# Zeroing the output in sixteen parts behind the load of expert 0's rows, an end flag read one double sooner on VectorE, and expert counts in four products

## The reference

```
scores = (z @ z^T) / S;  attn = relu(scores)^2;  x = u * (attn @ v)      B=8, S=3072, d=256, d_qk=64
logits = x @ w_gate;     expert = argmax(logits);  gate = softmax(logits)[expert]      E=8
each expert keeps its first 768 rows, in the order of the rows
h = relu(x_kept @ w1[expert]);  y = h @ w2[expert];  out[row] = gate * y   (rows not kept: 0)
```

## Time and profile before

| | |
|---|---|
| time, median of 3 runs | 877.05 us (876.01 to 877.35) |
| the profiled execution: its time | 877.52 us |
| its span in the profile | 875.7 us |
| around the span (877.52 - 875.7) | 1.8 us |
| groups 1 to 18, first to last logits product | 62.1 to 612.9 us |
| experts, first product to last scatter | 620.2 to 875.7 us |
| busy: TensorE, VectorE, ScalarE, GpSimd | 858.0, 635.4, 573.9, 123.4 us |

### The profile page before, as it was taken

One profiled execution on the slowest core, in us unless ns is written; L12 is line 12 of the kernel. 1 busy time (PEld: TensorE's weight loads), 2 busy tenths in 40 slices (PEclk: granted clock), 3 DMA queues, 4 the chain that ended last, 5 costly groups with the idle time before them and its releaser, 6 DMA issues.

```text
span 875.7 us, 22817 instructions
## 1 busy us (share of the span) xinstructions
PE 858.0 (98%) x7293; PEld 684.7 (78%) x7294; DVE 635.4 (73%) x1381; ACT 573.9 (66%) x874; POOL 123.4 (14%) x121
## 2 busy tenths in 40 slices
PE   6999999999999989999999999999999999999997
PEld 5887887888888867888888888888677777777776
DVE  7976777888888968878988888687564654655531
ACT  7968786768768668787868778678344434434422
POOL 0001102202201101102101110110112122221212
PEclk9999999999999999999999999999999999999999
DMA  7934636636733761210220220621635235324101
GB/s 274 363 103 149 206 89 231 203 104 220 216 112 104 248 188 32 72 44 28 72 54 24 66 60 23 232 60 24 109 113 160 72 107 168 119 67 150 54 18 36
DMA packets 127669, 104.52 MB, mean 119 GB/s; under 512 B 90541, under 2 KB 115194, under 8 KB 126624
## 3 DMA queue, kind: packets, MB, share of 16 engines
q1 hardware_dynamic: 122752, 91.61, 34.9%
q0 software_dynamic: 4896, 12.64, 4.0%
HBM read 40.03 MB, written 44.93 MB: 97 GB/s over the span
## 4 chain that ended last, share of the span: by engine, by line
PE 89%; DMA 3%; issue 2%; DVE 2%; SPq 1%; ACT 1%; ACTq 0%; POOL 0%; DVEq 0%; POOLq 0%
PE O L664 15%; PE O L668 15%; PE O L666 15%; PE Sc L777 14%; PE Sc L629 8%; PE Sc L630 7%; PE O L800 3%; PE O L804 3%; PE O L802 3%; PE M L804 2%; PE M L802 2%; PE M L800 2%; DMA rawv<-in_v 1%; DMA x<-disp 1%; SPq L266 1%
## 5 line engine op out<-in xcount | busy, mean ns | idle before, releaser
L664 PE MATMUL O<-vS,attn_hi 128*128 128x256 f16 x1332 | 363.5, 273 | 0.5 <-DVE vS L918 0.5
L666 PE MATMUL O<-vS,attn_hi 128*128 128x256 f16 x1332 | 363.4, 273 | 0.0
L668 PE MATMUL O<-vS,attn_lo 128*128 128x256 f16 x1332 | 363.3, 273 | 0.0
L451 ACT ACTIVATE Sc<-Sc 128x768 f32<-128x768 f32 x224 | 178.0, 795 | 93.2 <-PE Sc L630 72.8
L935 DVE TENSOR_TENSOR attn_lo<-attn,attn_hi 128x768 f16<-128x768 f32 x224 | 214.7, 958 | 7.7
L455 ACT ACTIVATE attn<-Sc 128x768 f32<-128x768 f32 x224 | 181.5, 810 | 7.1
L664 PEld LDWEIGHTS O<-vS,attn_hi 128*128 128x128 f16 x1332 | 130.4, 98 | 28.3 <-DVE ubuf L974 0.9
L666 PEld LDWEIGHTS O<-vS,attn_hi 128*128 128x128 f16 x1332 | 130.4, 98 | 26.7 <-issue 0.2
L629 PE MATMUL Sc<-zP 128*128 (+1 forms) x450 | 146.9, 327 | 4.0 <-issue 1.7
L929 DVE CAST attn_hi<-attn 128x768 f16<-128x768 f32 x224 | 124.8, 557 | 33.0 <-ACT attn L455 29.8
L630 PE MATMUL Sc<-zQ,zP 128*128 (+1 forms) x450 | 146.8, 327 | 0.0
(11 more groups left out here) (156 smaller groups left out, 916.9 us busy)
## 6 DMA issues: line engine op xcount, KB each, us to landing
out<-empty SPq DMA_DIRECT2D x8, 3072.0 KB, 11.5
wraw<-in_moe_w SPq DMA_DIRECT2D x16, 1024.0 KB, 7.1
rawv<-in_v SPq DMA_DIRECT2D x14, 768.0 KB, 8.2
ubuf<-in_u SPq DMA_DIRECT2D x19, 384.0 KB, 3.1
disp<-vS SPq DMA_DIRECT2D x8, 774.0 KB, 8.7
rawz<-in_z SPq DMA_DIRECT2D x3, 768.0 KB, 5.5
xT<-xrow SPq DMA_TRANSPOSE x54, 2.4
disp<-xrow,slot POOLq DMA_INDIRECT x54, 3.6
```

The lines of the kernel that those rows point to most:

```text
L451: act.activation(pair, pair, ACT.Relu).then_inc(s["relu_done"], 1)
L664: nc.tensor.matmul(o_part(t), hi, v[:, 0:D], start=c == 0 and j == 0 and t % 2 == 0, stop=False, skip_group_check=True)
L666: nc.tensor.matmul(o_part(t), hi, v[:, D:2 * D], start=False, stop=False, skip_group_check=True)
L668: ins = nc.tensor.matmul(o_part(t), lo, v[:, 0:D], start=False, stop=c == PAIRS - 1 and j == 1, skip_group_check=True)
```

## The change

It does three things. (1) `zero_out` leaves its place ahead of the weights' load and is issued in bodies 1 to 16 behind the transposed load of `x0` and ahead of the wait for it; each of its DMAs now covers a sixteenth of the output (1.5 MB). (2) VectorE reads the end flag after double 4 instead of after double 5; the other engines read it where they did. (3) `onehot` has a fourth tile, which is zeroed once; the totals come out of the same accumulation as the ranks, as its fourth tile, so that four products take the place of six, the first with 32 columns instead of 24.

```diff
--- before.py
+++ after.py
@@ -38,6 +38,7 @@
 AFTER_C = ROOT_C * ROOT_C
 FAR = 1 << 24
 FILL_ROWS = 6
+ZERO_PIECES = 16
 BLANK_AT = CHUNK + CHUNK // 2
 
 
@@ -110,7 +111,7 @@
         exsum = sb("exsum", [P, TILES], F32)
         key = sb("key", [P, TILES, E], F32)
         kmax = sb("kmax", [P, TILES], F32)
-        onehot = sb("onehot", [P, TILES, E], F16)
+        onehot = sb("onehot", [P, TILES + 1, E], F16)
         base = sb("base", [P, 2, E], F32)
         limit = sb("limit", [P, E], F32)
         over = sb("over", [P, E], F32)
@@ -229,11 +230,11 @@
             wait_apart(eng, s["flag_ready"], n)
             eng.reg_load(end, ends[0:1, bass.ds((n - 1) & (NG - 1), 1)])
 
-        def both_parts(eng, n, end, part, leave=None):
-
-            part(0, END_AT + 1)
+        def both_parts(eng, n, end, part, leave=None, at=END_AT):
+
+            part(0, at + 1)
             load_end(eng, n, end)
-            only_if(eng, True if isinstance(n, int) else eng.snap(end) > 0, lambda: part(END_AT + 1, PAIRS))
+            only_if(eng, True if isinstance(n, int) else eng.snap(end) > 0, lambda: part(at + 1, PAIRS))
             if leave is not None and not isinstance(n, int):
                 with eng.Else():
                     leave()
@@ -295,14 +296,6 @@
                                      ).then_inc(s["disp_filled"], 16)
                 only_if(sp, g == 0, load_batch)
                 if not isinstance(n, int):
-                    def zero_out():
-
-                        rows = B * S // 8
-                        sp.dma_start(out[bass.ds(((n - 1) & 7) * rows, rows), :].rearrange("(p r) d -> p r d", p=P),
-                                     empty[:, 0:D].unsqueeze(1).to_broadcast([P, rows // P, D])
-                                     ).then_inc(s["out_zeroed"], 16)
-                    only_if(sp, n <= 8, zero_out)
-                if not isinstance(n, int):
                     only_if(sp, n == 3, lambda: load_expert(0, 0))
                     only_if(sp, n == 5, lambda: load_expert(1, 1))
                 wait_apart(sp, s["loaded_u"], n * 16 + 16)
@@ -313,6 +306,13 @@
                     wait_apart(sp, s["scattered"], sp.snap(due))
                     sp.reg_mov(due, n * 48)
                     sp.dma_start_transpose(x0[:, :, :], disp_halves[0:GROUP, 0:2 * D]).then_inc(s["loaded_early"], 16)
+                    def zero_out():
+
+                        rows = B * S // ZERO_PIECES
+                        sp.dma_start(out[bass.ds(((n - 1) & (ZERO_PIECES - 1)) * rows, rows), :].rearrange("(p r) d -> p r d", p=P),
+                                     empty[:, :].unsqueeze(1).to_broadcast([P, rows // P, D])
+                                     ).then_inc(s["out_zeroed"], 16)
+                    only_if(sp, n <= ZERO_PIECES, zero_out)
                     wait_apart(sp, s["loaded_early"], n * 16)
                 load_end(sp, n, end)
             due = sp.alloc_register("due_SP")
@@ -388,7 +388,7 @@
                 only_if(pool, pool.snap(end) > 0, rest)
             attention_loop(pool, body)
             pool.drain()
-            pool.wait_ge(s["out_zeroed"], 16 * 8)
+            pool.wait_ge(s["out_zeroed"], 16 * ZERO_PIECES)
 
             with pool.Fori(0, E // 2) as i:
                 for k in range(4):
@@ -708,17 +708,15 @@
                                 ins.then_inc(s["logits_ready"], 1)
                             if not peeled and (c, t) == COUNTS_AT:
                                 pe.wait_ge(s["onehot_ready"], n)
-                                oh = onehot[:, :, :].rearrange("p t e -> p (t e)")
-                                counts = M[1][:, 0:TILES * E].rearrange("p (t e) -> p t e", t=TILES)
-                                nc.tensor.matmul(M[1][:, 0:TILES * E], before[:, :], oh, start=True, stop=False,
+
+                                counts = M[1][:, 0:(TILES + 1) * E].rearrange("p (t e) -> p t e", t=TILES + 1)
+                                nc.tensor.matmul(M[1][:, 0:(TILES + 1) * E], before[:, :],
+                                                 onehot[:, :, :].rearrange("p t e -> p (t e)"), start=True, stop=False,
                                                  skip_group_check=True)
-                                for k in range(TILES - 1):
-                                    nc.tensor.matmul(counts[:, k + 1:TILES, :], ones[:, :],
-                                                     onehot[:, k:k + 1, :].to_broadcast([P, TILES - 1 - k, E]),
-                                                     start=False, stop=k == TILES - 2, skip_group_check=True)
                                 for k in range(TILES):
-                                    ins = nc.tensor.matmul(M[1][:, 32:32 + E], ones[:, :], onehot[:, k, :],
-                                                           start=k == 0, stop=k == TILES - 1)
+                                    ins = nc.tensor.matmul(counts[:, k + 1:TILES + 1, :], ones[:, :],
+                                                           onehot[:, k:k + 1, :].to_broadcast([P, TILES - k, E]),
+                                                           start=False, stop=k == TILES - 1, skip_group_check=True)
                                 ins.then_inc(s["counts_ready"], 1)
                         if peeled and c == 0:
                             scores(K0 + LEAD, n, LEAD, par)
@@ -852,6 +850,7 @@
                 dve.memset(rank[:, :, e:e + 1], float(E - e))
                 dve.memset(base[:, 0, e:e + 1], float(e * capacity))
                 dve.memset(limit[:, e:e + 1], float((e + 1) * capacity))
+            dve.memset(onehot[:, TILES, :], 0.0)
             dve.memset(onesb[:, :], 1.0)
             dve.memset(ones[:, :], 1.0).then_inc(consts, 1)
 
@@ -1079,7 +1078,7 @@
                             route(dve.scalar_tensor_tensor(out=key[:, :, :], in0=below[:, :, :], scalar=0.0,
                                                            in1=rank[:, :, :], op0=ALU.is_ge, op1=ALU.mult))
                             route(dve.tensor_reduce(kmax[:, :], key[:, :, :], AX.X, ALU.max))
-                            dve.tensor_tensor(onehot[:, :, :], key[:, :, :], over_experts(kmax), ALU.is_equal
+                            dve.tensor_tensor(onehot[:, 0:TILES, :], key[:, :, :], over_experts(kmax), ALU.is_equal
                                               ).then_inc(s["onehot_ready"], 1)
                         if not peeled and c == ROUTE_AT[1]:
 
@@ -1095,7 +1094,7 @@
 
                             def over_tiles(x):
                                 return x.unsqueeze(1).to_broadcast([P, TILES, E])
-                            dve.tensor_tensor(base[:, 1, :], base[:, 0, :], M[1][:, 32:32 + E], ALU.add)
+                            dve.tensor_tensor(base[:, 1, :], base[:, 0, :], M[1][:, TILES * E:(TILES + 1) * E], ALU.add)
                             route(dve.tensor_tensor(posf[:, :, :], counts, over_tiles(base[:, 0, :]), ALU.add))
                             dve.tensor_tensor(over[:, :], base[:, 1, :], limit[:, :], ALU.subtract)
                             route(dve.tensor_tensor(fullp[:, :, :], posf[:, :, :], over_tiles(limit[:, :]), ALU.is_ge))
@@ -1105,7 +1104,7 @@
                             dve.tensor_scalar(ends[0:1, bass.ds((n - 1) & (NG - 1), 1)], least[0:1, :],
                                               0.0, float(NG + 1), ALU.is_lt, ALU.mult
                                               ).then_inc(s["flag_ready"], 1)
-                            route(dve.tensor_tensor(posf[:, :, :], posf[:, :, :], onehot[:, :, :], ALU.mult))
+                            route(dve.tensor_tensor(posf[:, :, :], posf[:, :, :], onehot[:, 0:TILES, :], ALU.mult))
                             dve.tensor_reduce(slot[:, :], posf[:, :, :], AX.X, ALU.max).then_inc(s["slot_ready"], 1)
                             dve.tensor_copy(base[:, 0, :], base[:, 1, :])
                             assert rs[0] == ROUTE_STEPS, rs[0]
@@ -1179,7 +1178,7 @@
                                 prep(z_fourth(), 4)
                                 prep(factor(), 5)
                         only_if(dve, g == 3, group3)
-                both_parts(dve, n, end, part)
+                both_parts(dve, n, end, part, at=END_AT - 1)
 
             PREP_STEPS = 5
```

## The result

The changed kernel takes 869.82 us (median of 4 runs, 869.65 to 870.06) where the kernel before took 876.59 in the same rounds (876.01 to 877.35): the ratio is 0.992, with a 95% interval of 0.9905 to 0.994. It is 6.8 us faster; forecast were 8.5. The profiled execution took 869.84 us against 877.52, 7.7 us less.

A forecast was written before the change was run, and what follows sets the result against it. TensorE's unbroken products were taken as the bound, with 7.7 us of excess in groups 1 to 9. Gains 3.3 + 2.5 + 1.4 + 0.4 + 1.0 - 0.1 = 8.5 us gave 868.5 from the 877.05 median; range 867.2 to 872.3.

The forecast's parts named there:

- The zeroing behind expert 0's rows: Attention, moved zeroing: TensorE's stop before group 9's logits goes (2.5 us), group 9 regains 1.4, groups 1 to 7 3.3.
- the floor of a group: Groups 10 to 17, TensorE busy without a pause: 31.94 us each, against which other groups' excesses, 7.7 us, were counted.
- The first rival: Group 8's piece delays expert 0's rows or group 9's transposes, giving back up to 3.9 us: 872.4; chance 0.08.
- The second: Groups 1 to 7: slow flag reads are not the zeroing's doing or stay slow, 3.3 us remain: 871.8; chance 0.07.
- The third: Groups 9 to 15: pieces catch TensorE's and ScalarE's flag reads, 0.5 us a group, 3.3 us back: 871.8; chance 0.06.
- The slower rival: Pieces push back the next group's transposes, 3.9 us per late group, 895.8 with all of groups 1 to 7; chance 0.03.
- One sign: GpSimd's end-flag reads in groups 9 to 16 would take about 0.9 us.
- The 1.4 us of group 9: Group 9: 1.4 of its 1.8 us excess returns without the clock's fall; 0.4 stays for another stop.
- The memset: Preamble: the extra memset, ahead of the one TensorE waits for, costs up to 0.06 us, taken as 0.1.
- The end of attention: Attention's end: VectorE 1.5 us sooner, SyncE then last and not moving, so 0.3 to 0.5 us gained, 0.4 taken.
- The count products: Every group, on TensorE: two fewer count products save 0.053 us in each of 18 groups, 1.0 us in all.
- the sum's own bounds: Whole kernel: the summed forecast could lie from 867.4 to 869.9 us, the upper with counts worth nothing and attention's end 0.3.

The follow-up runs named there:

- the run at the old place: The changed kernel with its sixteen zeroing pieces issued ahead of expert 0's rows, where the zeroing stood before: 876.26 us, ratio 1.000 to the kernel before.
- even a full part: The changed kernel with eight full zeroing parts in groups 1 to 8 instead of sixteen halves, at the new place: 869.88 us, ratio 0.9925 to the kernel before.
- the looks: Two further profiled executions of the kernel before, without any edit: 875.07 us and 877.10 us.
- the 46 runs: Runs of the unedited kernel before beside the experiments: 31 with mean clock 0.999 or more, median 875.7 us; 15 with 0.998 or less, median 877.3 us.
- the second look: The later of two further profiled executions of the kernel before, without any edit: 877.10 us.
- the count products alone: The kernel before with only the four count products and the memset they need: 875.49 us, ratio 0.9997 to the kernel before.

## Why the prediction was right, and where it was off

The direction, the mechanism and the range were right, and the time was 1.3 us above the forecast of 868.5.

The zeroing behind expert 0's rows: right in both effects. In group 8 2.6 us against 2.5; the split rows are late next, and in time. In groups 1 to 7 3.1 us (without the counts) against 3.3. The 31.94 us that the prediction took as the floor of a group is a mean with group 11 in it; without a pause most groups of the kernel before take 31.83. Groups 1 to 7 have such a longer group too, so their excess came out nearly right. The first rival (the piece gets in the way) is out by twice the size: even a full part does not. The second (the flag reads are not the zeroing's doing) is out by the placements: slow reads follow the zeroing from SBUF to wherever it is put, and stay fast when it is read from DRAM. The third (the pieces catch the reads of groups 9 to 15) did not happen, TensorE's longest there is 0.32 us; its price shows in the run at the old place, where groups 9 to 15 take 3.4 us more and the rival said 3.3. The slower rival, transposes pushed back, happened in no run with the new place. One sign did not come as written: GpSimd's reads of groups 9 to 16 were to be 0.9 us, and are 0.46 and 0.37 in groups 9 and 12 and 0.30 in group 16.

The Trainium skill (SBUF — State Buffer, the section on the two separate sides) has the rule that engine ports and DMA ports cannot contend. Applied to the register reads of this kernel it fails, and the measurements decide: they go from 0.30 to 0.94 us while a DMA reads SBUF. Which way such a read takes to SBUF, no trace shows. On the Trainium skill's DMA: Bandwidth & Descriptors (Queues, rings and completion order): the load of expert 0, with a piece right behind it, keeps 3.6 us where it took 9.97 behind a full part, as the ring order says.

The 1.3 us between forecast and measurement are 0.5 and 0.8. The 0.5 is the step from the profiled execution to the median. The sum was read off one execution of 877.52 us, which gave 869.0, and the same 0.5 us by which that execution lay above the median of before were then taken off again. But those 0.5 came from the stop and the fall of the clock, which the change removes: that execution had the fall and the longest stop of the three traces of before, and the changed kernel's runs lie within 0.4 us, the profiled one at 869.84 beside a median of 869.82. The same holds for the gain. The 1.4 us of group 9 are right for that execution and too much for the median of before, because the looks and the 46 runs show 1.6 us between executions with the fall and without, and a median that lies among those without. Three runs of before, 876.01 beside 877.05 and 877.35, already showed the two heights, and the mean clock of 0.998 in the profile was the hint. Against executions of before without the fall (875.7) the gain is 5.9 us, against those with it (877.3) 7.5.

The 0.8 is against the profiled execution, 869.0 forecast and 869.84 measured, and lies in small terms. The memset was put at 0.1 and costs 0.24 to 0.29 us, because it delays VectorE's chain in the preamble by more than its own length. The end of attention gives 0.15, not 0.4, because SyncE came 0.3 us later, relative to the last logits, than in the profile before: 0.2 of it lies ahead of the issue of expert 0's rows (2.81 us behind the logits, before 2.60), where it waits for `u`, and the rest behind it; `u` landed in 3.25 us and expert 0's rows in 3.62. The claim that SyncE "does not move" had no margin for the spread of two DMAs in a row. Groups 1 to 7 gave 0.25 less. The count products gave 0.05 us a group as forecast, 0.9 us in 18 groups where the sum had 1.0.

In the range, the upper of the sum's own bounds, 869.9, is 0.3 more than its two reasons give (868.5 and 1.0 for the counts and 0.1 for the end: 869.6), and the upper end of the range lies 0.1 below the 872.4 of the first rival. The measured time would have been inside either way.

## What to carry to other kernels

When a bulk store of constants or results can be issued at any time, put it behind the small loads that somebody waits for and behind the moment at which the engines read registers from SBUF; in this kernel its size mattered less than its place. A stop of TensorE has two prices, its own length and, in some executions, a stretch at half the clock: before a gain is read off one profile, compare its time and its mean clock with all the runs there are.

## What the runs showed of the hardware

A sequencer's read of a register from SBUF takes 0.26 to 0.33 us in most groups (0.49 to 0.56 in group 1), and mostly 0.85 to 0.98 us (1.4 at most) while a DMA reads zeros from SBUF. Batches and weights landing in SBUF (group 8: 0.30 us) and traffic from DRAM to DRAM (0.30) leave it alone. 1.5 MB of zeros took 6.4 us from SBUF and 10.7 from 128 KB in DRAM. Stops of TensorE of 2.0 to 2.4 us came with 3.41 us at 1.2 GHz in the three traces that had one of that length (the profile before, the second look, the count products alone); the fall began 0.25 us before the end of the stop in the first, and 0.75 and 0.96 us behind it in the others. In the one trace with a stop of 1.5 us the clock stayed full. There are no traces of the 46 runs, so how the length of the stop and the fall hang together stays open.
